# Attention stage of a fused attention and feed-forward kernel: transposes, copies and products one step later, another order of TensorE's and SyncE's work

## The reference

```
scores = q @ k.T / 8                                   # per batch and head
cum    = cumsum(max(s, 0))
scores = where(causal, -1e9, scores + min(-(cum_i - cum_j), 0))
attn   = softmax(scores)                               # with 1e-9 added to the sum
x      = (attn @ v) -> [2304, 512]
x      = rmsnorm(x) * g;  x = (silu(x @ w_gate) * (x @ w_val)) @ w_out     # 512 -> 1536 -> 512
h      = x @ w_in;        out = (h - tanh(h)) @ w_out2                     # 512 -> 2048 -> 512
```

## Time and profile before

| | us |
|---|---|
| median of 3 runs | 1107.17 (1105.19 to 1108.59) |
| the profiled execution, device time | 1106.37 |
| its span, first to last instruction | 1104.6 |
| attention stage, first score to first feed-forward product | 10.39 to 234.88 |

### The profile page before, as it was taken

How to read it: one execution, slowest core, us unless ns; L and a number is a source line. 1 busy time by engine, 2 the same in 40 slices (tenths; PEclk the granted TensorE clock), 3 DMA queues, 4 the chain that set the end, 5 groups by cost and what they waited for, 6 DMA issues and landing times.

```text
span 1104.6 us, 18165 instructions
## 1 busy us (share of the span) xinstructions
PE 1065.3 (96%) x6516; PEld 980.2 (89%) x6516; DVE 431.2 (39%) x1203; ACT 421.1 (38%) x1030; POOL 172.2 (16%) x184
## 2 busy tenths in 40 slices
PE   5888998899999999999999999999999999999998
PEld 4767777689999999999999999999999999999997
DVE  6656666654432222322322333533223232332322
ACT  5666677663431232222222233533223232322322
POOL 8767777640000000000000000000000000000000
PEclk9999999999999999999999999999999999999999
DMA  6555555322200000000000122210000000000000
GB/s 198 171 167 171 172 172 172 112 75 82 65 1 1 1 0 0 0 0 0 0 0 0 29 77 86 87 30 29 1 1 29 0 28 0 0 28 0 28 0 28
DMA packets 61251, 56.40 MB, mean 51 GB/s; under 512 B 7598, under 2 KB 51630, under 8 KB 61194
## 3 DMA queue, kind: packets, MB, share of 16 engines
q1 hardware_dynamic: 61194, 55.67, 16.5%
HBM read 41.63 MB, written 4.87 MB: 42 GB/s over the span
## 4 chain that ended last, share of the span: by engine, by line
PE 91%; DMA 2%; issue 2%; DVE 2%; POOL 1%; ACT 1%; SPq 0%; DVEq 0%; ACTq 0%; POOLq 0%
PE HP L958 15%; PE HP L960 15%; PE HP L959 15%; PE YP L959 11%; PE YP L960 11%; PE YP L958 11%; PE OP L927 5%; PE TP L911 4%; PE SC L896 3%; PE SC L897 2%; DMA RB<-PT 1%; DMA Qraw<-in_qT 1%; POOL KD L399 1%; DVE PR L675 1%; DVE PT L698 0%
## 5 line engine op out<-in xcount | busy, mean ns | idle before, releaser
L958 PE MATMUL HP<-XS,WA 128*128 128x384 f32 x576 | 194.6, 338 | 0.0
L960 PE MATMUL HP<-XS,WA 128*128 128x384 f32 x576 | 193.0, 335 | 0.0
L959 PE MATMUL HP<-XS,WA 128*128 128x384 f32 x576 | 192.7, 335 | 0.0
L777 DVE TENSOR_TENSOR AC<-AC,HP 128x384 f32<-128x384 f32 (+2 forms) x78 | 40.3, 522 | 293.4 <-PE HP L960 293.4
L828 DVE TENSOR_TENSOR AC<-HP,AC 128x384 f32<-128x384 f32 (+1 forms) x108 | 54.3, 512 | 216.3 <-ACT AC L603 216.3
L603 ACT ACTIVATE AC<-HP 128x384 f32<-128x384 f32 x96 | 47.2, 492 | 215.9 <-PE HP L960 215.4
L958 PEld LDWEIGHTS HP<-XS,WA 128*128 128x128 f32 x576 | 108.2, 188 | 2.6 <-issue 0.2
L959 PEld LDWEIGHTS HP<-XS,WA 128*128 128x128 f32 x576 | 108.2, 188 | 2.4
L911 PE MATMUL TP<-ident,PR 128*128 128x128 f32 (+1 forms) x480 | 86.8, 285 | 23.3 <-issue 16.6
L960 PEld LDWEIGHTS HP<-XS,WA 128*128 128x128 f32 x576 | 108.1, 188 | 0.0
L541 ACT ACTIVATE AC<-HP 128x384 f32<-128x384 f32 x72 | 35.4, 492 | 177.8 <-PE HP L960 177.8
(11 more groups left out here) (105 smaller groups left out, 1979.4 us busy)
## 6 DMA issues: line engine op xcount, KB each, us to landing
X<-in_w SPq DMA_DIRECT2D x52, 256.0 KB, 3.0
Kraw<-in_kT SPq DMA_DIRECT2D x16, 576.0 KB, 4.7
Qraw<-in_qT SPq DMA_DIRECT2D x16, 576.0 KB, 5.7
out_rows<-OS SPq DMA_DIRECT2D x18, 256.0 KB, 2.2
QO<-QA SPq DMA_DIRECT2D x15, 288.0 KB, 3.4
Vt<-in_v SPq DMA_DIRECT2D x16, 256.0 KB, 3.0
WRAW<-in_w SPq DMA_DIRECT2D x16, 256.0 KB, 4.3
RB<-PT SPq DMA_DIRECT2D x128, 32.0 KB, 2.2
```

Source lines behind the costliest of these rows:

```text
L777: dve.tensor_tensor(AC[:, m % 2, cols], AC[:, m % 2, cols], HP[:, 1, cols], ALU.mult).then_inc(prod_done if part is None else prod_part, 1)
L958: pe.matmul(dst, w(0), x(0), start=start, stop=False)
L959: pe.matmul(dst, w(0), x(1), start=False, stop=False)
L960: return pe.matmul(dst, w(1), x(0), start=False, stop=stop)
```

## The change

Transposes, copies, products and outputs come one step later (`T_LAG`, `V_LAG`, `O_LAG` from 2, 3, 4 to 3, 4, 5); `output` goes to the end of VectorE's step; TensorE makes both heads' scores first, then both heads' transposes; PR gets a fourth buffer; in SyncE's queue `load_qk` goes from u = 1 to u = 0, ahead of that step's RB, `load_qo` ahead of the RB of its step, and `load_v` from u = 3 to u = 4; the mean square comes one step later; the tail after the last step is written out anew.

```diff
-T_LAG, V_LAG, O_LAG = 2, 3, 4
+T_LAG, V_LAG, O_LAG = 3, 4, 5
-SQ_STEPS, MS_STEP, ROOT_STEP = (0, 1, 2, QB), 8, 2 * QB
+SQ_STEPS, MS_STEP, ROOT_STEP = (0, 1, 2, QB), 9, 2 * QB
-        PR = sb("PR", [P, 3, 2, PAD + S], F32)
+        PR = sb("PR", [P, 4, 2, PAD + S], F32)
...
@@ SyncE
                 if u == 0 and k + 1 < B * PAIRS:
                     wait(sp, scores_done, 2 * QB * k)
                     load_decay(*at)
-                if n >= T_LAG:
-                    load_rb(n - T_LAG)
-                if u == 1 and k + 1 < B * PAIRS:
-                    sp.wait_ge(q_hi, 2 * (k + 2))
-                    load_qo(*at)
                     if k + 2 < B * PAIRS:
...
                         load_qk(*after, k % 2)
-                if u == 3 and k + 1 < B * PAIRS:
-                    wait(sp, pv_done, QB * k)
-                    load_v(*at, (k + 1) % 2)
+                if u == 1 and k + 1 < B * PAIRS:
+                    sp.wait_ge(q_hi, 2 * (k + 2))
+                    load_qo(*at)
+                if n >= T_LAG:
+                    load_rb(n - T_LAG)
                 if u == 2 and 0 < k < B * PAIRS - 1:
                     sp.wait_ge(w_lo, k)
                     load_weights(*at)
+                if u == 4 and k + 1 < B * PAIRS:
+                    wait(sp, pv_done, QB * k)
+                    load_v(*at, (k + 1) % 2)
@@ VectorE
-                wait(dve, t_done, b * NG + groups_of(n - 3, 1)[-1][0] + 1)
+                wait(dve, t_done, b * NG + groups_of(n - 4, 1)[-1][0] + 1)
...
-                        if hh == 0:
-                            if n >= 1 or not first:
-                                recip(b, n - 1)
-                            if n >= O_LAG or not first:
-                                output(b, n - O_LAG)
+                        if hh == 0 and (n >= 1 or not first):
+                            recip(b, n - 1)
                         if n >= T_LAG or not first:
                             evacuate(b, n - T_LAG, hh)
...
+                    if n >= O_LAG or not first:
+                        output(b, n - O_LAG)
@@ TensorE
-                    if n >= T_LAG or not first:
-                        transposes(b, n - T_LAG, 0)
                     scores(b, n, 1)
...
                     if n >= T_LAG or not first:
-                        transposes(b, n - T_LAG, 1)
+                        for hh in range(2):
+                            transposes(b, n - T_LAG, hh)
                     if n >= V_LAG or not first:
                         values(b, n - V_LAG)
@@ TensorE, after the last step
             for hh in range(2):
-                transposes(B, -2, hh)
+                transposes(B, -3, hh)
+            values(B, -4)
             pe.wait_ge(mins_done, 2 * B * STEPS)
             pe.wait_ge(w_lo, B * PAIRS)
             gate(0, 0)
+            for hh in range(2):
+                transposes(B, -2, hh)
             values(B, -3)
+            value(0, 0)
             for hh in range(2):
                 transposes(B, -1, hh)
-            value(0, 0)
             values(B, -2)
             values(B, -1)
```

More of the change, by code:

```diff
@@ L458, in exponential @@
                 _, z, nk, _ = q_block(n % QB)
-                pr = PR[0:z, (b * STEPS + n) % 3, hh, PAD:PAD + nk]
+                pr = PR[0:z, n % 4, hh, PAD:PAD + nk]
                 act.wait_ge(mins_done, b * 2 * STEPS + 2 * n + hh + 1)
@@ L481, in pad @@
                 act.wait_ge(recip_done, b * STEPS + n + 1)
-                act.activation(PR[0:z, (b * STEPS + n) % 3, :, 0:PAD], RR[0:z, n % 4].rearrange("p (h o) -> p h o", o=1).broadcast_to([z, 2, PAD]), ACT.Copy
+                act.activation(PR[0:z, n % 4, :, 0:PAD], RR[0:z, n % 4].rearrange("p (h o) -> p h o", o=1).broadcast_to([z, 2, PAD]), ACT.Copy
                                ).then_inc(pad_done, 1)
@@ L674, in minima @@
                 end = S - P + z
-                dve.tensor_tensor_reduce(PR[0:z, (b * STEPS + n) % 3, hh, PAD:PAD + nk].rearrange("p (a f) -> p a f", a=halves), sc,
+                dve.tensor_tensor_reduce(PR[0:z, n % 4, hh, PAD:PAD + nk].rearrange("p (a f) -> p a f", a=halves), sc,
                                          mask[0:z, end - nk:end].rearrange("p (a f) -> p a f", a=halves),
@@ L911, in transposes @@
                         last = pe.transpose(TP[:, g % 2, i * P:i * P + z],
-                                            PR[0:z, (b * STEPS + n) % 3, hh, j * P:(j + 1) * P], ident[0:z, 0:z])
+                                            PR[0:z, n % 4, hh, j * P:(j + 1) * P], ident[0:z, 0:z])
                     last.then_inc(t_done, 1)
```

## The result

The changed kernel is slower: 1144.96 us (median of 4 runs, 1140.71 to 1149.88) against 1107.24, ratio 1.034 with a 95% interval of 1.030 to 1.039. The forecast was 1099, the range 1091 to 1108. The profiled execution took 1143.69 us with a span of 1141.9, so the span grew by 37.3 us.

The account below looks back on a forecast made before the run. It took a loop through RB's DMA in SyncE's queue to bound the attention pairs (13.77 us). Gains 8.0 + 0.8 + 0.6 + 0.3 less 0.3 and 0.8 gave 8.6, taken as 8: 1099 us, range 1091 to 1108.

Parts of the forecast that it names:

- a loop through SyncE's queue: Attention pairs: late RB delays VectorE's copy, TensorE's transposes and the next Q issue; its length sets 13.77 us a pair.
- the copies of u = 4: VectorE's half of the bank copies comes earlier, as `output` no longer stands before it; counted within +0.2 us net.
- the new wait at u = 0: TensorE's second-head transposes wait for bank 1, copied by VectorE at the end of step 4: 0.35 us a pair (0 to 0.5).
- quiet pair: TensorE's five steps of one attention pair, before any stall from RB: 12.95 us (12.5 to 13.2).
- the 5 + 5 blocks: Transposes of u = 4, where ScalarE must copy bank 0 between heads: known wait 0.21 us, +0.2 net (0 to 0.5).
- RB: the step that failed: RB of u = 2 lands at u0 + 9.4 (9.0 to 11.1); TensorE stalls 0 to 0.2 us, pair 13.1 us.
- rival 1: The loop only changes place: RB lands 6.1 us after Q, 13.8 us a pair, 1106 to 1107 us; chance 0.2.
- Rival 2: Slower: RB lands 7.0 us after Q or SyncE is as late; 14.7 us a pair, 1116 us; chance 0.12.
- Its wait for Q: GpSimd's wait, 2.32 us in the pair shown: goes or becomes waits for the scores; worth nothing.
- root pair: Pair k = 14, where table loads and the root stop ScalarE: from 16.85 to 16.2 us, gain 0.6.
- pairs k = 13 and 15: Special attention pairs: k = 13, with the mean square, from 15.64 to 14.8 us, gain 0.8; k = 15 gain 0.3.
- 0.14 for slower: Chance given to the whole changed kernel measuring slower, beside 0.66 for faster and 0.2 for the same.

Follow-up runs that it names:

- e12: The kernel before with only `output` moved to the end of VectorE's step, lags 2, 3, 4 kept: 1090.8 us, ratio 0.984 to the kernel before.
- e1: The changed kernel with SyncE's queue in the old order, all else as changed: 1091.61 us, ratio 0.984 to the kernel before.
- e6: The changed kernel with V issued at u = 3 as before instead of u = 4: 1107 us, ratio 0.997 to the kernel before.
- e5: The changed kernel with the QO copy cut to 4 of its 64 partitions: 1123 us, ratio 1.011 to the kernel before.
- e9: The kernel before with the lags 3, 4, 5 alone, `output` still in the middle of VectorE's step: 1108.2 us, ratio 0.999.
- e13: The changed kernel with K and Q issued at u = 1 behind QO, ahead of that step's RB: 1114.85 us, ratio 1.006 to the kernel before.
- e8: The changed kernel with V issued at u = 3 and QO cut to 4 of 64 partitions: 1093.12 us, ratio 0.985 to the kernel before.

## Why the prediction was wrong

**What bounds the kernel: right, but half read.** The 13.9 us of waiting for RB were the cause of most of TensorE's 16.6 (in e12 4.3 are left). I called it a loop through SyncE's queue and took its remedy to be the queue and the lag. The other half stood in the same two rows: a copy stood behind `output` on VectorE. Moving that alone (e12) is worth 17 us, as much as any version here gained; the prediction counted the move as a help to the copies of u = 4 only.

**TensorE's steps and the new wait at u = 0: about right.** The quiet pair was put at 12.95 us (12.5 to 13.2); e1, in which almost no RB wait is left, has 12.58. The new wait of 0.35 us was 0.30, the one at the 5 + 5 blocks 0.41 as 0.21 + 0.2 gave. The surplus lay in the steps that I counted without waits. (The terms as written add up to 12.90, or to 13.10 with the 0.2 us; the 12.95 is neither, which changes nothing here.)

**RB: the step that failed.** The prediction put V, KD, K, Q and RB in the right places, at nearly the right times, named the path (`output` of u = 2, then the products of u = 4 through OP's two buffers), and then took RB to be with VectorE 5.3 us after Q's issue, bounds 4.9 to 7.0. Over the twelve such waits in k = 2 to 13 it was 7.4 to 9.3 us, mean 8.5; the pair shown is the longest. I subtracted QO for no longer standing ahead, and added nothing for V now standing ahead and QO coming behind. e6 and e5 put these at 1.5 and 1.3 us on Q's median. They are rough: in the five experiments with the old queue order (e1 and e9 to e12) that median alone is 5.7 to 6.4 us. The bounds were the spread of one queue order, used for another.

The Trainium skill ("DMA: Bandwidth & Descriptors", section on queues, rings and completion order), which the prediction weighed, says that each DMA engine takes the descriptors of one issuing engine's row in ring order. That a small transfer then cannot pass a large one is the prediction's own conclusion; the section itself warns that completion is "not FIFO per issuing engine", since a later transfer can use fewer DMA engines than an earlier one. Here the conclusion held: RB came 0.3 us after Q in e13 too. The prediction gave it to rival 1 only as a question of place.

**Rival 2 was the case, with its size wrong.** Same mechanism, same place; its price was 14.7 us a pair and 1116 us. The waiting it named came out as 13 us over twelve pairs, about what it said (11). Nearly all of the other 22 us were the clock. The row was at hand: an idle time of 2.17 us had brought the granted clock to 0.50. Rival 2's own figures make TensorE wait about 1.75 us a pair (products at 11.55 instead of 9.8 us), and the price of a slow clock after it was left out. The runs give no limit below which it can be: waits of 1.81 and 1.86 us in the kernel before were followed by 1.00, but one of 1.46 us in e5 by 0.50. By the Trainium skill's page "TensorE: Matmul & The Clock Gate", part 1, activity is what releases the throttle, and idle time brings it back; the trace agrees, with 0.50 in 134 to 138 us after 4.0 us of idle time.

**GpSimd and SyncE.** Its wait for Q fell to 1.8 us in all, as said, and was worth nothing, as said. The root pair took 15.50 us instead of the forecast 16.2. The pairs k = 13 and 15, for which gains of 0.8 and 0.3 us were forecast, grew by 2.7 and 1.4. None of this matters beside the rest.

**The chances.** 0.14 for slower was too low for a queue order that puts a small, soon needed DMA behind two large ones, when no row showed V, K, Q and QO together. The range ended at 1108, 8 us below rival 2's own 1116; it should have held it.

**Open.** Why a transfer issued 2.3 us behind Q (QO) lengthens Q's own landing is not settled: only that taking it away shortens it. In the pair shown the DMA engines were 91 to 94% busy at 196 to 200 GB/s in 128 to 132 us, where they moved 393 GB/s over 144 to 146 us in the kernel before, while Q was under way there:

```profile
144.00:146.00 2.00, 2.00 (x17) 1.72 (x16) 1.97 (x9) 1.75 (x6) 0.79 (x1) 1.00 1.01 393
```

With QO cut to 18 KB (e5, e8), every stretch of 2 us in 100 to 150 us with 0.9 or more busy moved at least 251 GB/s. That points to the QO copy as the slow work; why it is slow, and whether WRAW (256 KB, issued at about 130 us) has a part, isn't shown. A third buffer for OP, which would have told the path through the products from that through ScalarE's copies, wasn't tried.

## What to carry to other kernels

An instruction that waits for a DMA belongs behind the work on its engine that others wait for; try that first, since here it brought the whole gain and no lag or queue order was needed. When a load is moved in a queue, price the landing of everything small behind it with all that is issued within a landing time on either side, not with the landing it had in the old order. And where a case leaves TensorE idle for about as long as a row of yours shows ahead of a slow clock, add that clock to its price: here it was the larger part, some 20 us against 13.

## What the runs showed that was not expected

- The median landing of one 576 KB load was 5.5 us in e8 and 7.8 us in the changed kernel, with the load itself unchanged and only its neighbours different: 288 KB closer ahead of it and 288 KB behind it. A copy issued behind a load lengthened its landing.
- For six pairs in a row, slow clock and DMA wait alternate (15 and 19 us). The reading that the slow pair hides the burst and the next one runs into it fits the rows and isn't tested.
- The same total of waiting on VectorE (21.4 and 21.7 us, e8 and e13) went with times 22 us apart.
- Lags 3, 4, 5 alone changed nothing (ratio 0.999), although VectorE's waits for RB fell from 13.9 to 7.9 us.
